# TensorE's order in every other tile: the second layer ahead of the turn and of the product with the values

## The reference

```python
B, H, S, D = q.shape                                    # 2, 8, 576, 64
scores = scale * np.matmul(q, k.transpose(0, 1, 3, 2))
kth = np.partition(scores, -32, axis=-1)[..., -32:-31]
scores = np.where(scores >= kth, scores, -1e9)
attn = softmax(scores)                                  # written out in the reference
x = (attn @ v) laid out as (1152 tokens, 512)
h = x @ w_in                                            # 512 -> 2048
g = np.maximum(h, 0.0) + alpha * np.minimum(h, 0.0)
x2 = g @ w_out                                          # 2048 -> 512
# then: gates of x2 (two small products), the best two of 8 experts for each token,
# out = sum over the two of weight * (relu(x2 @ w1[e]) @ w2[e])
```

## Time and profile before

| | us |
|---|---|
| median of three runs | 750.88 |
| the profiled execution | 749.59 |
| its span, first to last instruction | 747.8 |
| PE busy | 668.8 (89%) |
| DVE busy | 523.9 (70%) |
| ACT busy | 466.9 (62%) |
| POOL busy | 395.8 (53%) |

### The profile page before, as it was taken

One profiled execution on the slowest core, in us unless ns is written; L12 is line 12 of the kernel. 1 busy time (PEld: TensorE's weight loads), 2 busy tenths in 40 slices (PEclk: granted clock), 3 DMA queues, 4 the chain that ended last, 5 costly groups with the idle time before them and its releaser, 6 DMA issues.

```text
span 747.8 us, 13738 instructions
## 1 busy us (share of the span) xinstructions
PE 668.8 (89%) x4688; PEld 569.8 (76%) x4688; DVE 523.9 (70%) x1109; ACT 466.9 (62%) x880; POOL 395.8 (53%) x439
## 2 busy tenths in 40 slices
PE   2368777999989999999999988789999999999993
PEld 2256656887867888888888767688998989989992
DVE  5799997988769989898999134665554555555510
ACT  5588866777887787777777546624454553544511
POOL 3488799788788677777877735320220202202112
PEclk9956979999999999999999999879999999999997
DMA  9759436644507535254643749635827639357212
GB/s 293 332 181 413 124 164 241 247 164 155 209 17 264 194 128 208 99 230 157 235 160 124 277 187 362 240 104 185 262 86 246 176 119 295 107 188 238 71 24 35
DMA packets 39964, 141.01 MB, mean 189 GB/s; under 512 B 11152, under 2 KB 12176, under 8 KB 35856
## 3 DMA queue, kind: packets, MB, share of 16 engines
q1 hardware_dynamic: 35520, 130.25, 48.5%
q0 software_dynamic: 4384, 9.98, 6.0%
HBM read 113.70 MB, written 45.73 MB: 213 GB/s over the span
## 4 chain that ended last, share of the span: by engine, by line
PE 69%; POOL 12%; DMA 5%; issue 5%; ACT 4%; DVE 4%; SPq 0%; POOLq 0%; ACTq 0%; DVEq 0%
PE bank L1232 12%; PE bank L1057 10%; PE ps_scores L1216 9%; PE bank L1018 6%; PE bank L1216 6%; PE bank L995 6%; PE bank L1237 4%; PE ps_scores L948 3%; PE bank L1023 3%; POOL expo L1685 3%; PE bank L979 3%; DMA q_raw<-q_rows_dram 2%; DMA x_sorted_dram<-x,slot_i 2%; DVE top L438 2%; PE bank L1035 2%
## 5 line engine op out<-in xcount | busy, mean ns | idle before, releaser
L438 DVE MAX8 top<-rest 128x8 f32<-128x576 f32 x216 | 152.3, 747 | 0.0
L1840 POOL DMA_INDIRECT out_dram<-ye,xe x24 | 42.5, 1772 | 194.2 <-ACT ye L1597 189.4
L1685 POOL TENSOR_TENSOR expo<-scores,expo 128x576 f32<-128x576 f32 x72 | 103.8, 1442 | 64.4 <-ACT scores L1298 64.2
L450 DVE MATCH_REPLACE8 rest<-top,rest 128x576 f32<-128x576 f32 x144 | 105.8, 742 | 0.0
L1057 PE MATMUL bank<-w_out_high,g_parts 128*128 128x512 f32 x288 | 100.2, 410 | 0.0
L1232 PE MATMUL bank<-w_hi,he_t 128*128 128x512 f32 x256 | 91.9, 400 | 0.0
L655 DVE TENSOR_TENSOR w_lo<-raw,w_hi 128x1024 fp32r<-128x1024 f32 x64 | 77.9, 1225 | 18.9 <-ACT w_hi L1522 18.0
L995 PEld LDWEIGHTS bank<-v,prob_t 128*64 128x64 f32 (+1 forms) x1440 | 58.3, 147 | 29.5 <-ACT prob_t L1325 14.5
L995 PE MATMUL bank<-v,prob_t 128*64 128x65 f32 (+1 forms) x1440 | 74.0, 243 | 4.9 <-ACT prob_t L1325 4.9
L438 DVE MAX8 top<-scores 128x8 f32<-128x576 f32 x72 | 52.6, 747 | 31.2 <-ACT scores L1264 30.8
L948 PE MATMUL ps_scores<-k_parts,q_high 128*128 128x288 f32 (+1 forms) x160 | 56.0, 365 | 18.1 <-DVE q_low L495 7.9
(11 more groups left out here) (220 smaller groups left out, 1624.8 us busy)
## 6 DMA issues: line engine op xcount, KB each, us to landing
w_in_parts<-w_parts_dram SPq DMA_DIRECT2D x16, 2048.0 KB, 7.9
raw<-w_dram SPq DMA_DIRECT2D x64, 512.0 KB, 11.3
x_sorted_dram<-x_sorted_dram SPq DMA_DIRECT2D x7, 2570.0 KB, 10.8
w_parts_dram<-w_in_parts SPq DMA_DIRECT2D x4, 2048.0 KB, 9.9
q_raw<-q_rows_dram SPq DMA_DIRECT2D x18, 256.0 KB, 4.6
w_in_raw<-w_in_dram SPq DMA_DIRECT2D x4, 1024.0 KB, 11.2
w_out_raw<-w_out_dram SPq DMA_DIRECT2D x4, 1024.0 KB, 16.1
xe<-x_sorted_dram SPq DMA_DIRECT2D x7, 514.0 KB, 4.5
```

Source lines behind the costliest of these rows:

```text
L438: nc.vector.max(dst, src).then_inc(chain if r < ROUNDS - 1 else dve_top, 1)
L450: nc.vector.match_replace(rest[:, k, :], top[:, (n + k) % 4, 8 * r:8 * r + 8], src, LOWEST).then_inc(chain, 1)
L1685: nc.gpsimd.tensor_tensor(expo[:, n % 4, :], scores[:, n % SBUFS, :], expo[:, n % 4, :], ALU.mult).then_inc(pool_prob, 1)
```

## The change

In h = 2, 4 and 6 the call of `second_layer` stands ahead of `h_transpose` and `prob_values`. In h = 0 nothing moves. The other engines' programs are the same.

```diff
--- before.py
+++ after.py
@@ -1087,15 +1087,17 @@
                         h_transpose(blk - 2, REST_TURN_AT[h])
                     if mlp and h == 1:
                         x_transpose(blk - 1)
+                    if mlp and h in SECOND_AT:
+                        second_layer(blk - 1, SECOND_AT[h])
+                    if rest and h and h in REST_SECOND_AT:
+                        second_layer(blk - 2, REST_SECOND_AT[h])
                     if mlp and h in TURN_AT:
                         h_transpose(blk - 1, TURN_AT[h])
                     if h % 2 == 0 or h == 1:
                         prob_values(tile, h, blk, mixed_block, b)
                     if mlp and h in FIRST_AT:
                         first_layer(blk - 1, FIRST_AT[h])
-                    if mlp and h in SECOND_AT:
-                        second_layer(blk - 1, SECOND_AT[h])
-                    if rest and h in REST_SECOND_AT:
+                    if rest and h == 0 and h in REST_SECOND_AT:
                         second_layer(blk - 2, REST_SECOND_AT[h])
                     if h % 2 and h != 1:
                         prob_values(tile, h, blk, mixed_block, b)
```

## The result

The changed kernel took 755.35 us (median of 11 runs, 751.57 to 758.72), the kernel before 750.40 on the same chip (11 runs, 746.90 to 752.19): a ratio of 1.0064, with a 95% interval of 1.0042 to 1.0086. It is slower by 4.95 us (by the interval, 3.2 to 6.5), and the forecast was 4.0 more and 754.9, with a range of 752.2 to 759. The profiled execution took 754.76 us (span 753.0) against 749.59 (747.8).

What follows compares the result with a forecast made beforehand. TensorE was taken to bound the attention part from block 4 on. Third tile -0.5, fifth -2.9, seventh +6.2 and block 3 +1.2 gave +4.0 us on the 750.88 median: 754.9 us, range 752.2 to 759.

Steps and rivals of the forecast that it cites:

- TensorE bounds the stretch, so a wait counts in full: Attention part from block 4 on: TensorE sets the time, so a wait added or removed counts in full.
- Seventh tile: h = 6: second layer waits 0.94 us for ScalarE's copy of the transposed block; +6.2 us over six blocks without block 3.
- the counter's way, some 0.05: Seventh tile: about 0.05 us from the end of ScalarE's copy (294.73) until the second layer can start (294.78).
- Third tile: h = 2, blocks 2 to 8: second layer's first weight load no longer open; 0.08 us less each, -0.5 us in all.
- Fifth tile: h = 4, blocks 2 to 8: the turn no longer waits for ScalarE's copy of the chunk; -2.9 us in all.
- The thin cover: Third and fifth tiles: despite ScalarE's lateness, GpSimd's product stays hidden from TensorE by 0.3 us or a little more.
- rival 3: Fourth and sixth tiles: the 0.3 us cover is missing, GpSimd's products come late; 4.2 us over fourteen tiles, 759.1 us; 14%.
- Block 3: ScalarE's lateness from the fifth tile lasts into the seventh, wait about 2.1 us, partly given back; +1.2 us, bounds 0 and 2.1.
- Rival 1: Seventh tiles: the wait for the transposed block never binds, only gains are left; 746.9 us; 6%.
- Rival 2: Blocks 2 and 3 wait for ScalarE and GpSimd anyway, so the loss is partly absorbed; +2.1 us, 753.0 us; 17%.
- Rival 4: Seventh tiles: TensorE's clock falls behind the new wait, +11 us if in all seven, 766 us; 4%.

Runs made afterwards that it cites:

- e2: Kernel before, with the second layer moved ahead in the seventh tile alone: 756.15 us, ratio 1.0068 to the kernel before.
- e3: Changed kernel, with ScalarE's copy of the transposed block ahead of its two prob_t copies in the seventh tile: 747.93 us, ratio 0.9954 to the kernel before.
- e5: Changed kernel, except that block 3's fifth tile keeps the second layer behind the product: 754.47 us, one execution.
- e7: Changed kernel, with ScalarE's relu_both behind the two exponentials in third, fifth and seventh tiles: 753.78 us, one execution.
- e8: Changed kernel with the edits of e3 and e7 together: 746.65 us, ratio 0.9947 to the kernel before.
- e1: Changed kernel, with the seventh tile's second layer put back behind turn and product (move in third and fifth tiles alone): 748.01 us, ratio 0.9961 to the kernel before.
- e6: Changed kernel, with ScalarE's copy of the transposed block one instruction later, behind the cast high_g: 771.03 us, ratio 1.0259 to the kernel before.
- e4: Kernel before, with only ScalarE's early copy of the transposed block in the seventh tile: 751.22 us, ratio 0.9997 to the kernel before.

## Why the prediction was right, step by step

**TensorE bounds the stretch, so a wait counts in full.** Right outside block 3: the tiles' lengths give 4.97 us where the medians differ by 4.95 (interval 3.2 to 6.5), and e2 and e3 moved the time by what they did to one wait. In block 3 a wait of 0.7 us costs nothing (e2, e5, e7).

**Seventh tile.** Right in mechanism, a tenth short in size. Foretold were a wait of 0.94 and a second layer 2.02 behind the tile's start; measured 0.88 and 2.12. The step that was off is "the counter's way, some 0.05": from the end of the copy (299.23) to the first matmul (299.38) it is 0.15. TensorE's weight load at that place, after:

```profile
299.35 0.19 PEld L1057 LDWEIGHTS bank<-w_out_high,g_parts 128*128 128x128 f32 x1 [1.08 <-issue]
```

It starts at 299.35, 0.12 behind the end of the copy, and not ahead of the wait. By the Trainium skill (TensorE: Matmul & The Clock Gate, "Step-by-step: what each phase is for") a weight load may be pulled ahead of matmuls in front of it. In this trace it was not pulled ahead of the wait for its own matmul's data. The layer takes 2.84 us from its first matmul here and 2.76 in e8, where it follows the scores, so the open load costs at least 0.08 in each tile. The 0.05 that I took holds at another place. ScalarE's copy of a chunk and TensorE's weight load for its turn, before, at the wait of the earlier trace rows:

```profile
431.93 0.60 ACT L1354 COPY h_sb<-bank 128x512 f32<-128x512 f32 x1
432.58 0.42 PEld L1035 LDWEIGHTS bank<-ident,h_sb 128*128 128x128 f32 x4 [1.26 <-ACT h_sb L1354]
```

There the load and the matmul both start 0.05 behind the copy's end (432.53 to 432.58). Both ways run from ScalarE to TensorE with a load that lies open, so the open load alone does not explain the other 0.10; why the way is longer ahead of the second layer stays open. So +1.12 in place of +1.03 in five blocks. Block 8 has +1.23 in place of +1.09, with a wait of 1.41; 0.05 of that comes with the late product of the sixth tile (below), since e2 and e7 have 7.28 and 7.29 us there instead of 7.33. In sum that is +6.8 where I had +6.2.

**Third tile.** -0.3 in place of -0.5. In blocks 4 to 7 third and fourth tile together are 0.05 to 0.09 shorter, as computed (0.08). Block 3 gave 0.01, and block 8 lost 0.07 net, on which below.

**Fifth tile.** -2.6 in place of -2.9. Blocks 2 to 7 as foretold: 0.21, 0.05, 0.88, 0.29, 0.30, 0.30 against 0.2, 0.1, 0.9, 0.3, 0.3, 0.3. Block 8 gave 0.60 and not 0.8. e1 shows that these gains stand alone.

**The thin cover (rival 3).** In block 6 the cover was sized right, though two of its terms were off: ScalarE waits until 4.60 us behind the third tile's start, 1.83 later than before where I had 1.70, and the next `prob_t` copy is 0.92 late where I had 0.75. GpSimd's product for the fifth tile of block 6, after:

```profile
328.81 1.44 POOL L1687 TENSOR_TENSOR expo<-scores,expo 128x576 f32<-128x576 f32 x1 [1.76 <-ACT scores L1300]
```

It ends at 330.25, and TensorE takes it at 330.52: 0.27 us of cover, where I had worked out 0.3. But I used block 6 for all blocks. In block 8 the fourth and sixth tiles have no scores, so they are half a microsecond shorter, and the cover was gone. GpSimd and TensorE there, after:

```profile
416.34 1.42 POOL L1687 TENSOR_TENSOR expo<-scores,expo 128x576 f32<-128x576 f32 x1 [2.42 <-ACT scores L1300]
```

```profile
413.32 0.66 PE L979 MATMUL bank<-ident,expo 128*128 128x128 f32 x4
...
416.78 0.95 PE L995 MATMUL bank<-v,prob_t 128*64 128x65 f32 x20
417.81 0.66 PE L979 MATMUL bank<-ident,expo 128*128 128x128 f32 x4
```

The product ends at 417.76 and the transposes start at 417.81, not right behind the product with the values: the tile takes 4.49 instead of 4.29. With the sixth tile (4.96 for 4.78) that is 0.4 us. Of this 0.1 is the lengthening that I had in the sum. So rival 3 exists, in two tiles of fourteen, and e7 takes its 0.28 back by letting the exponentials go first. My terms for block 8 together (-0.08 - 0.8 + 1.09) made +0.2; measured are +0.7.

**Block 3.** Right in its sum (+1.14 for +1.2) and in its cause, ScalarE's lateness out of the fifth tile, which e1, e2, e5 and e7 show from four sides: the loss is there without the seventh tile's move, and gone without the fifth tile's or with `relu_both` behind the exponentials. The wait was 1.89 (I said about 2.1). One step was wrong: I let the give-back come from the 1.39 us wait in block 4's first tile. That wait is still there, 1.41. TensorE, after:

```profile
211.70 0.64 PE L979 MATMUL bank<-ident,expo 128*128 128x128 f32 x4
...
220.64 0.66 PE L1035 MATMUL bank<-ident,h_sb 128*128 128x128 f32 x4 [1.41 <-ACT h_sb L1356]
```

What gave way is a wait for GpSimd's product at the start of block 4. Before, TensorE had this row there:

```profile
212.15 0.66 PE L979 MATMUL bank<-ident,expo 128*128 128x128 f32 x4 [0.74 <-POOL expo L1685]
```

After, the row at 211.70 has no wait. The seventh tile grew by 2.14, the eighth lost 0.82 and block 4's first 0.18. This is also why the seventh tile's own wait costs nothing in block 3 (e2, e5), and why removing it there gains nothing.

**The rivals.** Rival 1 (no wait) fell to the seven waits. Rival 2 (absorbed) was half true, for the waits in block 3 alone; block 2, which I had thrown in with it, lost its 0.8 in full. Rival 3 holds in two tiles. Rival 4 did not come: the clock was 1.00 over the whole stretch, behind all seven waits. In e6 it came behind waits of 1.98 us and more.

**The sum.** Foretold -0.5 - 2.9 + 6.2 + 1.2 = +4.0; in the trace -0.3 - 2.6 + 6.8 + 1.1 = +5.0. Every mis-sized term is small and all but block 3's have one sign: the gains came out smaller and the cost larger than foretold. The forecast of +4.0 stayed within the measured 3.2 to 6.5.

## What to carry to other kernels

When work is moved ahead on the bounding engine, find the last input of the moved step and read where its producer stands in the order of its own engine: here one copy, queued behind two that wait for the same tile, turned a gain of some 3 us into a loss of 5, and moving that copy (worth nothing by itself, e4) turned it back. Whatever is moved back in exchange, here the turn, delays not only its reader but all that is queued behind that reader, and this shows where that engine has no idle time left (block 3), or the cover was sized on a longer tile than the shortest one (block 8). So size a cover on the tile with the least work in it.

## What the runs showed of the hardware

**The same waits need not bring the same clock.** Before, waits of 1.12 and 1.27 us were followed by 4.44 us at a clock of 0.62. In the changed kernel the same two waits stand in the same place, and the clock stayed up. TensorE, after:

```profile
440.38 0.66 PE L1035 MATMUL bank<-ident,h_sb 128*128 128x128 f32 x4 [1.12 <-ACT h_sb L1356]
...
442.31 0.63 PE L1004 MATMUL bank<-ident,x 128*128 128x128 f32 x4 [1.27 <-ACT pos L1392]
```

and its busy time and clock in that stretch, and in block 2's second tile, after:

```profile
124.52:134.68 10.16, 8.50 (x45) 0.66 0.01 2
442.69:447.50 4.81, 4.81 (x24) 1.00 0.00 0
```

The other way round, block 2's second tile took 10.16 us at 0.66 there and 7.28 at full clock before:

```profile
124.56:131.84 7.28, 5.61 (x45) 1.00 0.01 2
```

That is 2.9 us in one place and 1.6 in the other, as large as most terms of this study. Of the ten profiled executions (before, after, e1 to e8) eight lost time in block 2's second tile, which took 8.8 to 10.3 us in them and 7.28 and 7.30 in the kernel before and in e8. Behind the two waits of 1.12 and 1.27 us the clock was 0.61 to 0.71 in seven, and 1.00 in the changed kernel, e1 and e2. e4, which has TensorE's order of the kernel before, had 0.61 for 7.3 us in block 2, so the fall there does not need the change. A difference of 3 us between single executions of this kernel says little by itself; the tiles of blocks 5 to 7 that an edit leaves alone repeat to 0.02.

**Falls behind single waits.** In e6 the clock was 0.50 in the second layer behind two of the five waits of 1.98 us (blocks 4 and 6, 1.6 us each) and behind those of 2.45 and 2.80 (blocks 3 and 8), and full behind the other three. Behind the change's own waits, of 0.88, 1.41 and 1.89 us, it stayed full. But behind the wait of 1.4 us in block 4's first tile it fell in e3 and e4 and in none of the other eight executions. So the length of the last wait does not decide it alone, and one execution of each kernel is too little for a rate.

**The way of a semaphore.** From ScalarE's end to the second layer's first matmul it is 0.15 us (299.23 to 299.38), from ScalarE's end to a turn 0.05 (432.53 to 432.58), and from GpSimd's end to the next transposes 0.05 (417.76 to 417.81). What makes the first longer is not shown.
